# At attention's end, seven PSUM copies move from ScalarE to VectorE, between the steps of the tile table

## What is computed

```python
def _attn_ref(q, kv, w_sr):                 # q (2, 12288, 128), kv (2, 384, 32, 128)
    kv_flat = mean of 4 x 4 cells of kv, @ w_sr      # 768 keys, also the values
    a = softmax(q @ kv_flat.T / sqrt(128))
    return a @ kv_flat

def _moe_ref(x, w_gate, w1, w2):            # 8 experts, 128 -> 1024 -> 128
    expert = argmax(x @ w_gate); gate = softmax(...)[expert]
    out[token] = gate * relu(x @ w1[expert]) @ w2[expert]

def _moe2_ref(x, expert_emb, tau, w1, w2):
    logits = normalised(x) @ normalised(expert_emb).T / tau     # otherwise as above
```

## Time and profile before

| what | us |
|---|---|
| median of three runs | 1861.44 (1859.93 to 1862.42) |
| the profiled execution: its own time | 1861.18 |
| the profiled execution: span of the trace | 1859.4 |
| TensorE busy | 1808.8 (97% of the span) |
| VectorE busy | 1414.6 (76%) |
| ScalarE busy | 1247.8 (67%) |
| GpSimd busy | 795.4 (43%) |

### The profile page before, as it was taken

How to read it: one execution, slowest core, us unless ns; L and a number is a source line. 1 busy time by engine, 2 the same in 40 slices (tenths; PEclk the granted TensorE clock), 3 DMA queues, 4 the chain that set the end, 5 groups by cost and what they waited for, 6 DMA issues and landing times. The chain is left out here.

```text
span 1859.4 us, 65000 instructions
## 1 busy us (share of the span) xinstructions
PE 1808.8 (97%) x18846; PEld 1629.1 (88%) x18847; DVE 1414.6 (76%) x3610; ACT 1247.8 (67%) x2907; POOL 795.4 (43%) x1120
## 2 busy tenths in 40 slices
PE   6899999999999999999999999999799999999998
PEld 5788888888888888889888888988699999999997
DVE  5789998889888537888888777777467777767676
ACT  1677777788887637777777777776355555555554
POOL 0033333367664523555455455544243333333333
PEclk9999999999999979999999999999899999999999
DMA  7022222233343221322322111111211111111110
GB/s 295 18 85 83 83 88 63 76 114 118 123 134 95 75 68 42 82 70 80 83 70 67 46 50 47 43 37 31 66 58 50 47 50 40 51 46 51 46 50 25
DMA packets 108829, 132.23 MB, mean 71 GB/s; under 512 B 16430, under 2 KB 86202, under 8 KB 108736
## 3 DMA queue, kind: packets, MB, share of 16 engines
q1 hardware_dynamic: 79232, 83.91, 16.2%
q0 software_dynamic: 19456, 38.20, 6.1%
q10 hardware_dynamic: 10048, 8.92, 1.7%
HBM read 90.41 MB, written 42.65 MB: 72 GB/s over the span
## 5 line engine op out<-in xcount | busy, mean ns | idle before, releaser
L1995 DVE SCALAR_TENSOR_TENSOR hT_l<-ps_hidden,hT_l 128x512 f16<-128x512 f32 x436 | 300.0, 688 | 126.9 <-ACT hT_l L1930 119.0
L2328 DVE SCALAR_TENSOR_TENSOR hT_l<-ps_hidden,hT_l 128x512 f16<-128x512 f32 x388 | 268.3, 691 | 161.4 <-ACT hT_l L2285 154.7
L2285 ACT ACTIVATE hT_l<-ps_hidden 128x512 f16<-128x512 f32 x388 | 231.6, 597 | 207.7 <-PE ps_hidden L2226 207.5
L1930 ACT ACTIVATE hT_l<-ps_hidden 128x512 f16<-128x512 f32 x436 | 260.2, 597 | 157.2 <-PE ps_hidden L1860 150.8
L1860 PE MATMUL ps_hidden<-xT_l,W 128*128 128x256 f16 x2616 | 358.1, 273 | 1.1 <-DVE xT_l L1990 1.1
L2367 POOL DMA_INDIRECT out<-out_rows_l,out_slots_l x194 | 188.4, 971 | 350.2 <-DVE out_rows_l L2336 311.5
L1875 PE MATMUL ps_y<-W,hT_l 128*128 x1744 | 323.9, 279 | 0.2 <-DVE hT_l L1995 0.2
L2226 PE MATMUL ps_hidden<-xT_l,W 128*128 128x256 f16 x2328 | 319.3, 274 | 1.0 <-DVE xT_l L2314 1.0
L1620 POOL DMA_INDIRECT rows<-grp_rows,grp_slots x210 | 210.0, 1000 | 184.3 <-ACT grp_rows L1564 59.3
L721 POOL DMA_INDIRECT rows<-att_rows,att_slots x192 | 189.7, 988 | 229.4 <-ACT exps L1264 90.3
L2240 PE MATMUL ps_y<-W,hT_l 128*128 x1552 | 276.6, 273 | 0.2 <-DVE hT_l L2328 0.2
(11 more groups left out here) (253 smaller groups left out, 2919.5 us busy)
## 6 DMA issues: line engine op xcount, KB each, us to landing
x_l<-rows SPq DMA_DIRECT2D x206, 130.0 KB, 2.1
w_chunk<-in_moe_w SPq DMA_DIRECT2D x34, 512.0 KB, 4.5
W<-in_kv SPq DMA_DIRECT2D x24, 512.0 KB, 13.0
q<-in_q SPq DMA_DIRECT2D x48, 256.0 KB
size_chunk<-in_moe_w SPq DMA_DIRECT2D x18, 512.0 KB, 4.0
w_chunk<-in_moe_w ACTq DMA_DIRECT2D x16, 512.0 KB, 3.9
rows<-grp_rows,grp_slots POOLq DMA_INDIRECT x210, 2.4
out<-out_rows_l,out_slots_l POOLq DMA_INDIRECT x194, 2.3
```

The lines of the kernel that those rows point to most:

```text
L1930: nc.scalar.activation(hT[:, p, 0, :], psH[:, (HP * h + p) % HB, :], ACT.Relu).then_inc(h_high, 1)
L1995: nc.vector.scalar_tensor_tensor(out=hT[:, p, 1, :], in0=psH[:, (HP * h + p) % HB, :], scalar=0.0, in1=hT[:, p, 0, :], op0=ALU.max, op1=AL ...
L2285: nc.scalar.activation(hT[:, p, 0, :], psH[:, p, :], ACT.Relu).then_inc(h_high, 1)
L2328: nc.vector.scalar_tensor_tensor(out=hT[:, p, 1, :], in0=psH[:, p, :], scalar=0.0, in1=hT[:, p, 0, :], op0=ALU.max, op1=ALU.subtract).then ...
```

## The change

The copies of units 9 to 15 leave ScalarE's list in body 51 and stand in VectorE's list of the same body (`vec_copy`, a `tensor_copy` with the same waits, and one more so that `copied` is counted in order). The 17 table steps from `pads` to `wexp` also move into VectorE's body 51, between these copies; only `rows` stays behind the pipeline. `pads` now stands ahead of the first copy and ahead of `slot_1`; three copies (9, 10, 11) stand ahead of `slot_1`, four behind it. `vec_make` becomes `vec(dve, *names)`; every step now waits for the step before instead of for itself. The second table, after the first experts, has the same steps at its old place.

```diff
+    def vec_copy(self, dve, i):
+        dve.wait_ge(self.turned, i + 1)
+        dve.wait_ge(self.copied, i)
+        wait(dve, self.made, i - 1)
+        self.nc.vector.tensor_copy(self.copy[i % 2], self.turn[i % 2]).then_inc(self.copied, 1)
...
-    def vec_make(self, dve):
...
+    def vec(self, dve, *names):
+        nc, k, v = self.nc, self.k, self.nc.vector
         nxt = k.next_slot[:, self.layer, :]
...
+        for name in names:
+            self.steps.wait_before(dve, 0, name)
+            if name == "pads":
+                ins = v.tensor_copy(self.pads[:], nxt)
...
+            else:
+                dve.wait_ge(self.in_rows, 1)
+                ins = v.tensor_copy(k.tiles[:, self.layer], self.turned.rearrange("p (w t) -> p w t", w=2))
+            self.steps.did(name, ins)
...
                 if isinstance(t, int) and t == QT + 3:
-                    for i in range(9, gates.UNITS):
-                        gates.act_copy(act, i)
                     gates.act_gates(act)
...
                     low_q(t + 1, 1 - par)
+                finishing = isinstance(t, int) and t == QT + 3
+                if finishing:
+                    table.vec(dve, "pads")
+                    gates.vec_copy(dve, 9)
+                    table.vec(dve, "count", "up", "int")
+                    gates.vec_copy(dve, 10)
+                    table.vec(dve, "shifted", "tiles")
+                    gates.vec_copy(dve, 11)
                 route((), ("slot_1",))
+                if finishing:
+                    gates.vec_copy(dve, 12)
+                    table.vec(dve, "left", "steps", "ends")
+                    gates.vec_copy(dve, 13)
+                    table.vec(dve, "passed", "expert", "gone")
+                    gates.vec_copy(dve, 14)
+                    table.vec(dve, "nth", "offset", "start")
+                    gates.vec_copy(dve, 15)
+                    table.vec(dve, "start_min", "wexp")
...
             pipeline(dve, body)
-            router.slotting.wait(dve, groups - 1)
-            table.vec_make(dve)
+            table.vec(dve, "rows")
...
-            table.vec_make(dve)
+            table.vec(dve, *table.STEPS)
```

More of the change, by code:

```diff
@@ L895, in __init__ @@
         self.in_rows = ctx.enter_context(nc.semaphore(f"{name}_in_rows"))
-    def vec_make(self, dve):
-        nc, k, st = self.nc, self.k, self.steps
+    def vec(self, dve, *names):
+        nc, k, v = self.nc, self.k, self.nc.vector
         nxt = k.next_slot[:, self.layer, :]
[L901 to L928, removed]
```

36 lines of the change are left out of this document (added).

## The result

The changed kernel took 1850.21 us (median of four, 1849.21 to 1852.87) against 1861.72 for the kernel before in the same comparison: ratio 0.9944, interval 0.9929 to 0.9959. The forecast was 1853.8 with a range from 1852.0 to 1859.0, so the sign and the mechanism at attention's end were right and the size was too small. The profiled execution took 1850.20, with a span of 1848.4 against 1859.4: 11.0 us less.

The account below looks back on a forecast made before the run. Bound at attention's end by ScalarE's late copy, then by TensorE's fallen clock. With the clock held, 8.3 less 0.7 gives 7.6 us: 1861.18 - 7.6 + 0.26 = 1853.8, range 1852.0 to 1859.0.

Parts of the forecast that it names:

- the mechanism at attention's end: Copies on VectorE shorten TensorE's stall at gate 9 and its clock stays up; 7.6 us gained, chance 0.50.
- The stall: TensorE's wait at gate 9 for copy 9: 3.3 us less, leaving about 0.5 of 3.8.
- The copy on VectorE: Each 128x512 copy from PSUM on VectorE takes 0.68 us, with 0.53 and 0.95 as ends.
- The clock held: Units after gate 9: PEclk stays 1.00, 1.47 us a step, gate 15 at 657.3, TensorE through 13 us earlier.
- The first rival: The clock falls all the same near 650, TensorE still ends the block; gain 4.3 us, 1857.1; chance 0.38.
- The bound behind it: At attention's end the last landing of the sends becomes the limit: 8.3 us net, 4.7 of TensorE's 13 becoming waiting.
- kept for the range: Earlier `pads` moves SyncE's fills forward and may bring the last landing up to 0.6 us forward; counted only in the bounds.
- The next block's start: After idling from 659.6 to 664.8, TensorE starts the next block at 1.2 GHz; costs 0 to 1.4 us, 0.7 taken.
- cold entry: Next block's idle matmuls start at 1.2 GHz after TensorE's idle time; 0.7 us charged.
- The sends: GpSimd's chain untouched, 0.97 us each; rivals had sends stretched in part (1857.9, chance 0.05) or beyond 0.84 (over 1862, 0.02).
- `slot_1` and the table steps: VectorE's list: steps between copies hide, 1.3 us a unit against TensorE's 1.47; `slot_1` may cost a few tenths, taken by slack.

Follow-up runs that it names:

- e10: The changed kernel without the four idle matmuls behind each of units 9 to 16; 1850.23 us, ratio to before 0.9949, near condition.
- e12: The kernel before with only the seven copies moved to VectorE, `pads` and the whole table staying behind the pipeline; 1857.50 us, ratio 0.9989, near condition.
- e11: The changed kernel, unchanged, run again in the near condition; 1852.96 us, ratio to before 0.9952.
- third group: Runs in the near condition: the changed kernel with and without its idle matmuls behind units 9 to 16, against before at 1860.06 us.
- e15: The changed kernel with only `pads` and the copies ahead, the table's other steps staying behind the pipeline; 1852.20 us, ratio to before 0.9956, near condition.
- e1: The changed kernel, unchanged, run again in the far condition; 1924.92 us against 1922.71 for before, ratio 1.0010.
- e7: The changed kernel, unchanged, run again in the far condition for its profile; ratio 1.0009 against before at 1929.93 us.
- the first and the third group: First: far condition, the changed kernel again and variants, before at 1922.71 us. Third: near condition, before at 1860.06 us.

## Why the prediction missed, point by point

- **The stall, right.** 3.3 us less stall were forecast: gate 9 starts 3.61 us earlier, and the stall is 0.23, not 0.5.
- **The copy on VectorE, right.** 0.68 taken from the nearest row, 0.69 measured, seven times. The estimate by the Trainium skill's table, 0.66 ("VectorE: DVE Perf Modes", section on the TRN2 errata), is 0.03 off.
- **The clock held, right in the near condition**, with gates at 1.47 to 1.48 and gate 15 at 657.09 (657.3 forecast). The first rival, at 0.38, had the clock fall all the same; that happened in e10, behind a stall of 0.42 us and with thinner work, and in every far trace.
- **The bound behind it, right.** The last landing ends the block; TensorE waits 4.0 (4.7 forecast). The term was 8.3 us and is 8.7: SyncE was through 2.4 us behind the start of the last send, not 2.9, most of the 0.6 that was "kept for the range". e12 shows that, once the copies are early, `pads` must be early too, worth 5 us, where the forecast gave them at most 0.6.
- **The next block's start, wrong by 0.6.** The forecast charged 0.7 us for a cold entry. After's entry was cold, as it said, but before's own was already one of the long ones, and little was added: 8.21 before, 8.27 after. The earlier trace rows had the clock at 0.91 there for a moment and I read that as a gain to be lost.
- **A term that was missing.** This is the step that failed: the sum ends at the next block's start, and everything behind it was put at nothing, without a reason, as if it moved as one piece. It doesn't: E, which holds the last experts' entry, came out 2.4 us shorter, F 0.6 shorter and D 0.7 longer, 2.3 us in all. Without these 2.3 the two errors above, 0.4 and 0.6, would have left the time near 1852.8, inside the range. Sum: 8.68 + 2.41 + 0.61 + 0.05 - 0.06 - 0.69 = 11.0. In e11's trace the same kernel gives 8.6. The range lacked some 2 us on either side for this. How far the median fell is in part luck: in the third group the changed kernel took 1852.96 against 1860.06, 7.1 us less where 7.6 was forecast.
- **The sends, right.** 971/972/1007 ns beside the copies, and the same without them. The Trainium skill's rule ("SBUF — State Buffer", "Who interferes with whom") agrees with the trace.
- **`slot_1` and the table steps, right.** The steps cost nothing (e15's B is 17.56, after's 17.67), and behind `slot_1` the gates stay 1.48 us apart.

That E and F go by chance and not by the change is shown in part. After's traces have E at 12.30 and 15.08, so 12.30 is not what the change always gives. F is 0.6 us longer in the two traces of before (537.75 and 537.81 against 537.10 to 537.17 in all seven others) because their first output matmuls still run at the low clock (0.64 us in the earlier trace rows, 0.39 in after). But the last experts' entry is long in all five traces of before, so a share of some 2 us that belongs to how before arrives there isn't excluded. Five traces of each kernel can't tell. What D's 0.7 in after are stays open too.

## What to carry to other kernels

Where an engine that is the bound does thin work, price a stall by the clock that it loses and not by its length: 3.8 us of standing still cost 8.7, and 60 idle matmuls in the gap gave back 7.6 in the trace. When the longest chain gets shorter, look for the smallest step that feeds the next one: with the copies early, the place of `pads`, 0.12 us of work, decided over 5 us, since an 8 us fill hangs on it. And before a forecast's range is closed, list every later place where the clock may rise or fall. Two such places were worth 1.3 and 2.3 us here in one and the same kernel (the changed one's first entry at 8.27 and 7.01, its last at 7.08 and 9.36), and a third some 2 us between kernels.

## What the runs showed of the hardware

- Every kernel has two conditions here, from group to group and not within one: near 1860 and near 1925 us. In the far one TensorE was idle 37 us more and busy 35 us more (85.3 and 1834.8 of 1920.1, e1, against 48.2 and 1800.2 of 1848.4, after), stalls without a releaser come on TensorE, VectorE and ScalarE, most often of 1.1 us on VectorE in the last experts (21 of the 25 in e7's line 2363) and up to 7.5 us at the longest. The cause of the condition is open. It isn't a matter of the chip alone: the first and the third group ran on the same chip.
- The clock's rise at the last experts' entry came 2.6 us behind the first idle matmuls in after and 9.2 us in e11, the same kernel (worked out from PEclk 0.80 in the window from 1306 and 0.63 in that from 1312). The Trainium skill ("TensorE: Matmul & The Clock Gate", Part 1) says that the window in which the chip watches TensorE runs freely and isn't reset when a kernel starts, and that the point of transition varies by 0.5 us to either side for that reason. That the point varies from run to run agrees with e11 against after; the 6.6 us between them are far more than the page gives for matmuls back to back, and for an entry, which has waits in it, the measurement decides.
- TensorE, busy without a gap in the profile from 652 to 658 us in both, ran at 0.50 in e10 and at 1.00 in after; the kernels differ in four idle matmuls a unit. After's clock fell too, near 658.3, still without a gap. A busy share near 1 in the windows doesn't say that the clock will hold. Each is one trace; e11 repeats after's (1.00 to 658, then 0.53), and nothing repeats e10's.
